# Two more banks for the first products of the last layer, and output products five steps behind instead of four

## The reference, cut to what matters

```python
def _moe2_ref(x, w_in, w_out, a, b):
    h = x @ w_in                      # 1152x512 @ 512x2048
    h2 = h * h
    h3 = h2 * h
    P = a[0] + a[1] * h + a[2] * h2 + a[3] * h3
    Q = 1.0 + np.abs(b[0]) * np.abs(h) + np.abs(b[1]) * h2
    g = P / (Q + 1e-06)
    return (g @ w_out).astype(np.float32)   # 1152x2048 @ 2048x512
```

## Time and profile before

| | |
|---|---|
| median of 3 runs | 810.62 us (808.42 to 811.71) |
| the profiled execution | 812.09 us |
| its span, first to last instruction | 810.4 us |
| mean granted TensorE clock | 0.958 |
| last layer, from the first `in_step` to the last matmul | 595.7 to 805.8 us |
| PE busy, whole span | 740.9 us (91%) |
| DVE, ACT, POOL busy | 81%, 61%, 44% |

### The profile page before, as it was taken

The page is one execution under the profiler, slowest core; times in us unless marked ns, Lnnn a source line. Parts: engine busy times, 40 slices in busy tenths (PEclk is TensorE's granted clock), DMA queues, the critical chain, the costliest instruction groups (busy, mean ns, idle before and its releaser), DMA issues.

```text
span 810.4 us, 15534 instructions
## 1 busy us (share of the span) xinstructions
PE 740.9 (91%) x5370; PEld 693.6 (86%) x5370; DVE 658.5 (81%) x1664; ACT 491.5 (61%) x890; POOL 359.8 (44%) x531
## 2 busy tenths in 40 slices
PE   5899999999999999847999999999469999999997
PEld 4788888898888888737999999999459998898996
DVE  3999899999999999925667667676649988888885
ACT  6677666666667776433444444554537767767773
POOL 4646465554558784240000000000049678666764
PEclk8799999999999999967999999999869999999999
DMA  9740000600000203022567576676811002000001
GB/s 191 170 149 14 1 16 1 221 4 13 14 2 15 105 2 105 1 117 59 210 171 251 172 235 214 185 209 185 242 39 40 1 1 79 0 1 15 26 1 39
DMA packets 61978, 71.20 MB, mean 88 GB/s; under 512 B 21969, under 2 KB 41937, under 8 KB 61906
## 3 DMA queue, kind: packets, MB, share of 16 engines
q1 hardware_dynamic: 60466, 65.57, 27.6%
q0 software_dynamic: 1440, 4.72, 1.7%
HBM read 56.12 MB, written 14.16 MB: 87 GB/s over the span
## 4 chain that ended last, share of the span: by engine, by line
PE 63%; DVE 21%; issue 5%; DMA 4%; ACT 3%; POOL 3%; SPq 1%; DVEq 0%; ACTq 0%; POOLq 0%
PE bank L1398 16%; PE bank L1399 16%; PE bank L1400 16%; DVE best L737 7%; DVE pairs L739 5%; PE bank L1304 4%; PE bank L1280 2%; PE bank L1270 2%; DVE best L758 2%; DVE pairs L720 2%; DVE pairs L756 2%; DMA slots_out<-y_blocks 2%; PE bank L1287 1%; PE bank L1256 1%; DMA k_rows<-in_k 1%
## 5 line engine op out<-in xcount | busy, mean ns | idle before, releaser
L955 DVE RECIPROCAL r<-c 128x384 f32<-128x384 f32 x48 | 122.5, 2552 | 25.1 <-POOL c L676 24.9
L1026 ACT ACTIVATE probsT<-bank 96x768 f32<-96x768 f32 x72 | 58.1, 807 | 99.5 <-PE bank L1287 99.5
L737 DVE MAX8 best<-pairs 128x8 f32<-128x288 f32 x288 | 116.0, 445 | 0.0
L665 POOL DMA_INDIRECT x_rows<-slots_out,slot_index x9 | 11.2, 1240 | 225.4 <-DMA slots_out<-y_blocks 223.9
L1304 PE MATMUL bank<-v_rows,probsT 96*128 96x65 f32 (+1 forms) x960 | 106.4, 264 | 3.8 <-ACT probsT L1026 3.3
L1304 PEld LDWEIGHTS bank<-v_rows,probsT 96*128 96x128 f32 (+1 forms) x960 | 102.0, 181 | 8.5 <-ACT probsT L1026 7.3
L884 DVE TENSOR_TENSOR wl<-raw,wh 128x1024 fp32r<-128x1024 f32 x72 | 87.1, 1217 | 19.9 <-ACT wh L1120 19.9
L739 DVE MATCH_REPLACE8 pairs<-best,pairs 128x288 f32<-128x288 f32 x216 | 94.8, 445 | 0.0
L1134 ACT ACTIVATE hTh<-bank 128x288 fp32r<-128x288 f32 x64 | 26.4, 413 | 104.4 <-PE bank L1400 104.4
L1398 PE MATMUL bank<-xTh,wh 128*128 128x288 f32 x256 | 76.6, 299 | 13.0 <-DVE xTl L896 13.0
L575 POOL TENSOR_TENSOR pairs<-scores 128x288 int32<-128x288 int32 x72 | 57.6, 801 | 67.5 <-ACT scores L1012 67.4
(11 more groups left out here) (138 smaller groups left out, 2144.1 us busy)
## 6 DMA issues: line engine op xcount, KB each, us to landing
raw<-in_moe_w SPq DMA_DIRECT2D x16, 2048.0 KB, 8.8
slots_in<-zeros SPq DMA_DIRECT2D x18, 256.0 KB
slot_rows<-slots_in SPq DMA_DIRECT2D x32, 144.0 KB, 8.7
slots_out<-y_blocks SPq DMA_DIRECT2D x32, 144.0 KB, 8.1
raw<-in_moe_w_in SPq DMA_DIRECT2D x8, 512.0 KB, 8.0
v_rows<-in_v SPq DMA_DIRECT2D x16, 144.0 KB, 4.4
out_rows<-out_rows SPq DMA_DIRECT2D x9, 256.0 KB, 2.3
q_rows<-in_q SPq DMA_DIRECT2D x8, 256.0 KB, 3.1
```

The lines of the kernel that those rows point to most:

```text
L737: ins = nc.vector.max(best, cur)
L955: nc.vector.reciprocal(rS[x][:], cS[x][:]).then_inc(s_d2, 1)
L1026: nc.scalar.activation(pT[x % 2][:], T_ps[0:KP, 0:KJ * P], ACT.Exp, scale=SCALE).then_inc(s_ex, 1)
```

## The change

`LAG` becomes 5, for all 48 steps. The steps 0 to 4 now write the banks 0, 1, 2, 6 and 7; from step 5 on the banks 0, 1 and 2 are taken in turn, beginning with 0. What an `in_step` waits for follows from that: steps 0 to 4 for no `g`, step 5 for `g` of step 0, step 6 for that of step 1, step 7 for that of step 2, and step 8 for that of step 5, since step 5 is the one that used bank 0 last. From there on it is again the `g` of three steps before. `rows_out` moves from `f` = 3 to `f` = 4 with `LAG`. No instruction is added or removed.

```diff
-LAG = 4
+LAG = 5
...
+        H2_FIRST = (0, 1, 2, 6, 7)
+
+        def h2_bank(m):
+            return bank(H2_FIRST[m] if m < len(H2_FIRST) else (m - len(H2_FIRST)) % 3)
+
+        def h2_steps_before(m):
+            return 0 if m < 5 else m - 4 if m < 8 else m - 2
...
-                hp = bank(m % 3)[:, 0:GN]
+                hp = h2_bank(m)[:, 0:GN]
...
-                if m >= 3:
-                    pe.wait_ge(s_g, m - 2)
+                if h2_steps_before(m):
+                    pe.wait_ge(s_g, h2_steps_before(m))
...
-                    last = product(bank(m % 3)[:, 0:GN], wh[sl][:, c:c + P], wl[sl][:, c:c + P],
+                    last = product(h2_bank(m)[:, 0:GN], wh[sl][:, c:c + P], wl[sl][:, c:c + P],
```

## The result

| | before | after |
|---|---|---|
| median of 16 runs each | 810.64 us (808.42 to 812.68) | 812.34 us (810.90 to 814.24) |
| ratio after / before | | 1.0025, 95% interval 1.0016 to 1.0033 |
| the profiled execution | 812.09 us | 812.40 us |
| its span | 810.4 us | 810.7 us |
| mean granted TensorE clock | 0.958 | 0.963 |

The change makes the kernel 2.0 us slower (0.25%, interval 1.3 to 2.7 us). That is within the 0.5% that was called no change, and with 16 runs on each side it is clear of zero. Every ratio here leaves out two single executions that ran far longer at a lower granted clock (854.70 us of the kernel before, 935.57 us of e11). The two profiled executions differ by less, because the stages ahead of the last layer, which the change does not touch, happened to take 2.4 us less in the one of after: step 0 begins at 593.36 instead of 595.74.

What follows compares the result with a forecast made beforehand. PE's own work was taken as the bound (740.9 of 810.4 us busy); +0.14 us up to step 9 and +1.99 us at the end, about +2.1 on the 810.62 us median, gave 812.7 us, range 810.0 to 815.2.

Steps and rivals of the forecast that it cites:

- The hole before step 3 goes, one before step 8 comes: PE's step loop: the 2.34 us idleness before step 3 vanishes; PE idles 4.43 us before step 8 instead.
- The chain does not speed up: Elementwise chain making `g`: earlier products find no one waiting, so `g` of step 5 stays at 625.01.
- Rival D: Chain of `g` speeds up with earlier products: +1.3 us, or -2.2 us if step 8 never waits; chance 0.05.
- Start of step 8: Step 8 waits for `g` of step 5 and starts at 625.06, 1.76 us ahead of the kernel before.
- The clock after the new wait: PE's clock falls again in the hole before step 8, losing 1.9 us, so step 9 starts +0.14 us later.
- A: The main case: step 8 waits and the clock loses 1.6 to 2.4 us, +1.8 to +2.6 us; chance 0.62.
- C: Rival, slower: clock stays at 1.2 GHz as from 592 to 599.5, losing 3.75 us, +4.0 us, 814.6; chance 0.20.
- The end: Six output steps instead of five follow the last input step, the last without waiting: +1.99 us.
- The sum: Whole kernel: 812.09 + 0.14 + 1.99 = 814.2 us as profiled; median forecast 812.7 us, no change that can be told.
- the old hole: Wait before step 3: costs 4.14 us in all, of which 1.65 us is step 3 running at slow clock.

Runs made afterwards that it cites:

- e11: The change's new banks with lag 4 and output step 4 issued before step 8; ratio to the kernel before 0.9963, last layer 207.44 us.
- e8: The changed kernel with POOL's three gathers in steps 5 to 7 instead of 1 to 3; ratio to before 1.0066, last layer 217.06 us.
- e9: The changed kernel with two output steps in step 9 and lag 4 from there on; ratio to before 1.0028, last layer 212.77 us.
- e3: The changed kernel with 24 extra matmuls, unused by the result, before step 8; ratio to before 1.0006, last layer 210.37 us.
- e4: The kernel before with 13 extra matmuls, unused by the result, before step 3; ratio to before 1.0000, last layer 210.03 us.
- e5: The changed kernel with its five banks kept through step 9, lag 4, next group's transposes in steps 11 to 14; ratio to before 0.9971, last layer 206.91 us.
- e7: The kernel before with only the next group's transposes moved from steps 8 to 11 to steps 11 to 14; ratio 1.0000, last layer 210.12 us.
- e6: The same bank order and moved transposes as e5, but with lag 5; ratio to before 1.0005, last layer 210.47 us.
- e1: The change's new banks with the old lag of 4; ratio to the kernel before 0.9971, last layer 208.38 us.
- e2: The kernel before with lag 5 and the old banks; ratio to before 1.0014, last layer 211.36 us.

## Why the prediction was right

- **The hole before step 3 goes, one before step 8 comes.** Forecast 4.43 us, ended by `g`; measured 4.37. From step 3's first matmul to step 9's it was 629.64 - 601.49 = 28.15 us, forecast 27.5; the difference is the clock, below.
- **The chain does not speed up.** Forecast 18.71 us from `g` of step 0 to that of step 5; measured 18.70. Rival D falls. e8 shows that something could have sped it up, the gathers, but not earlier products.
- **Start of step 8.** Forecast 625.06 - 595.74 = 29.32 us after step 0; measured 29.35.
- **The clock after the new wait.** Forecast 1.9 us, from slow phases of 3.4 and 4.1 us; measured 5.3 us of slow phase. Step 8 and output step 3 with the transposes took 629.64 - 622.71 = 6.93 us instead of 4.44, so 2.5 us. This term was 0.6 us too small, just above A's 1.6 to 2.4 us and well below C's 3.75. None of the rows read beforehand had so long a slow phase under a full load. C's row has none of 7.5 us either: step 0 starts at 595.74, and before it PE worked only in pieces, so its full load at half clock lasted 3.8 us. That the clock could fall inside the longer hole, 1.5 us before its end, was not considered; e9's 4.35 us hole was followed by 5.2 us of slow phase too. e3 confirms the size with 2.4 us.
- **The end.** Forecast +1.99 us and no wait at the last output step. In the sum that term is right: step 9 starts 0.76 us later after step 0 than before (36.28 against 35.52), the last layer is 2.68 us longer, and the 1.92 us that are added behind step 9 are the end. Its wording, that the end costs, invites a wrong reading: e9 takes the output step away from the end and gains nothing.
- **The sum.** +2.1 us forecast; +2.7 in the profile, of which 0.6 are the clock, and +2.0 (1.3 to 2.7) over the runs. The forecast of 812.7 us stands beside a median of 812.34. That the runs' +2.0 lies nearer to it than the profile's +2.7 is no merit of the sum, whose clock term was too small for the profile; so far it is luck.
- **What was wrong in the working and did not touch the result.** I priced the old hole at 4.14 us and its clock at 1.65 of them. The whole price was right, since the change reached the wait before step 8 6.1 us sooner, as summed; but e4 shows that the clock's share was covered by step 4's wait for `g` of step 1, and could not have been won alone. The kernel with the shortest last layer, e5, got 3.2 us of the 4.14.

The cause is settled as far as these runs go: both halves of the change work, in opposite directions. What is open is why the profiles give +2.7 and the runs +2.0. The last layer repeats well from profile to profile (210.12 in e7 against 210.10 before, 212.77 in e9 against 212.78), and the interval of the runs just reaches 2.7. A loss at the clock that is smaller in other executions would fit, as would e3's 1.5 us by the ratios against 2.4 in the profiles, but one profile of each kernel cannot show it.

## What to carry to other kernels

Where an engine runs its list in order, freeing one wait only helps up to the next one, so recompute every later wait with the new, earlier arrival: here step 8 was reached 6.1 us sooner and could start 1.7 us sooner. A larger lag between making and using did not give slack to the step that waits here; it took away the work that covered the wait. A slow clock behind a hole costs only if nothing else would have been waited for in that time, so fill the hole with useless work once and see, before pricing it.

## What the hardware did that I had not expected

The slow phase after a hole was not of one length under full load: 3.0 us behind 3.42 us of idleness (e8, step 8), 3.4 behind 2.34 (before, step 3), 4.1 behind 12.98 (before, at 370), 5.3 behind 4.37 (after, step 8). Nor does the clock fall at one point of a hole: in the change it fell 1.5 us before PE resumed, in the kernel before just as it did, and in e6 PE's first matmul behind the 2.15 us hole was shown 0.44 us long, near full speed, and the clock then read 0.74 and 0.50 in the two stretches from 658 to 662, while PE was working. In e1 a hole of 1.71 us left it at full speed. The Trainium skill, "TensorE: Matmul & The Clock Gate", Part 1, says that the moment of the change is independent of where the kernel's own work begins and so varies from run to run. The traces agree as far as they go: behind step 0, where the programs are still the same, the clock rose 3.8 us after its first matmul in the kernel before and 4.6 us after it in e2.
